# The last stage's first layer in 128 + 128 + 64 rows, with the 64-row products of both column halves on two row tiles

## The reference

```python
def _moe2_ref(x, w_in, w_out, g_ln):
    h = x @ w_in                                   # [1536, 320] @ [320, 1024]
    h_max = np.max(h, axis=-1, keepdims=True)
    e = np.exp(h - h_max)
    sm = e / (np.sum(e, axis=-1, keepdims=True) + 1e-09)
    solu = h * sm
    mu = np.mean(solu, axis=-1, keepdims=True)
    var = np.mean((solu - mu) ** 2, axis=-1, keepdims=True)
    ln = (solu - mu) / np.sqrt(var + 1e-06) * g_ln
    return (ln @ w_out).astype(np.float32)         # [1536, 1024] @ [1024, 320]
```

## Time and profile before

| | us |
|---|---|
| median of three runs | 579.95 (579.08 to 581.56) |
| the profiled execution's own time | 582.91 |
| its span, first to last instruction | 581.2 |
| TensorE busy in it | 538.9 (93%) |
| VectorE busy | 229.0 (39%) |
| ScalarE busy | 134.7 (23%) |
| mean granted TensorE clock | 0.977 |

### The profile page before, as it was taken

How to read it: one execution, slowest core, us unless ns; L and a number is a source line. 1 busy time by engine, 2 the same in 40 slices (tenths; PEclk the granted TensorE clock), 3 DMA queues, 4 the chain that set the end, 5 groups by cost and what they waited for, 6 DMA issues and landing times.

```text
span 581.2 us, 8810 instructions
## 1 busy us (share of the span) xinstructions
PE 538.9 (93%) x2735; PEld 364.8 (63%) x2736; DVE 229.0 (39%) x502; ACT 134.7 (23%) x283; POOL 100.0 (17%) x121
## 2 busy tenths in 40 slices
PE   2699994489999999999999999999998999999996
PEld 2688993366656666666656666666675465565654
DVE  6197886931121213121211212131102656556643
ACT  3435453001111111111111111111111223323222
POOL 2425540121011001100110110010006112213000
PEclk9999998589999999999999999999998999999999
DMA  5957853557777721101100111010062111111100
GB/s 169 285 166 236 240 177 117 182 177 249 235 230 219 224 107 50 38 23 38 50 25 25 50 38 35 26 50 11 23 203 81 34 34 45 56 34 47 33 23 23
DMA packets 32707, 59.68 MB, mean 103 GB/s; under 512 B 5536, under 2 KB 21888, under 8 KB 32560
## 3 DMA queue, kind: packets, MB, share of 16 engines
q1 hardware_dynamic: 24288, 42.28, 23.1%
q0 software_dynamic: 3136, 10.03, 6.2%
q10 hardware_dynamic: 5264, 7.12, 3.5%
HBM read 49.96 MB, written 9.45 MB: 102 GB/s over the span
## 4 chain that ended last, share of the span: by engine, by line
PE 86%; DVE 6%; DMA 3%; issue 2%; ACT 1%; SPq 1%; POOL 0%; DVEq 0%; POOLq 0%; ACTq 0%
PE ps_y L1134 23%; PE ps_a L1113 9%; PE ps_lr L1113 9%; PE ps_y L1185 8%; PE ps_a L1177 6%; PE ps_lr L1177 5%; PE ps_b L1123 5%; PE ps_y L1052 3%; PE ps_lr L1103 3%; PE ps_a L1103 2%; PE ps_t L1090 2%; PE ps_b L1194 2%; PE ps_a L1025 2%; PE ps_b L1034 1%; DMA mb_sb<-m_dram 1%
## 5 line engine op out<-in xcount | busy, mean ns | idle before, releaser
L1134 PE MATMUL ps_y<-w_sb,hT 128*128 x496 | 138.7, 433 | 0.5 <-DVE hT L859 0.5
L859 DVE COPY hT<-ps_b 128x512 f32<-128x512 f32 x86 | 55.4, 686 | 209.4 <-PE ps_b L1123 182.4
L1134 PEld LDWEIGHTS ps_y<-w_sb,hT 128*128 128x128 f32 x496 | 93.1, 190 | 42.8 <-issue 8.4
L475 POOL DMA_INDIRECT xg<-x_dram,token_idx x31 | 29.6, 955 | 245.1 <-PE ps_t L1090 240.2
L1113 PE MATMUL ps_a<-w_sb,xT 128*128 x128 | 57.7, 593 | 0.0
L1185 PE MATMUL ps_y<-wout_sb,hT 128*128 128x320 f32 x192 | 53.9, 433 | 1.9 <-DVE hT L859 1.9
L1113 PE MATMUL ps_lr<-w_sb,xT 128*128 x120 | 55.5, 605 | 0.0
L1185 PEld LDWEIGHTS ps_y<-wout_sb,hT 128*128 128x128 f32 x192 | 35.6, 190 | 16.1 <-DVE hT L859 2.4
L576 ACT COPY y_sb<-ps_y 128x320 f32<-128x320 f32 x31 | 13.2, 426 | 122.7 <-PE ps_y L1134 122.7
L1113 PEld LDWEIGHTS ps_lr<-w_sb,xT 128*128 128x128 f32 x120 | 21.6, 189 | 26.5 <-issue 26.5
L1113 PEld LDWEIGHTS ps_a<-w_sb,xT 128*128 128x128 f32 x128 | 23.1, 190 | 23.3 <-issue 23.3
(11 more groups left out here) (164 smaller groups left out, 559.3 us busy)
## 6 DMA issues: line engine op xcount, KB each, us to landing
w_sb<-w SPq DMA_DIRECT2D x8, 1280.0 KB, 6.2
w_sb<-w SPq DMA_DIRECT2D x16, 512.0 KB, 4.3
mb_sb<-m_dram SPq DMA_DIRECT2D x12, 512.0 KB
y_dram<-y_sb ACTq DMA_DIRECT2D x31, 160.0 KB, 1.8
kvo_sb<-kvo SPq DMA_DIRECT2D x12, 324.0 KB
qk_sb<-qk SPq DMA_DIRECT2D x24, 160.0 KB
w_sb<-w SPq DMA_DIRECT2D x16, 128.0 KB, 5.0
gate_o<-og ACTq DMA_DIRECT2D x1, 1920.0 KB, 7.6
```

The costliest lines, as they stand in the source:

```text
L475: pool.indirect_dma_start(out=xg[:, b % 2], out_offset=None, in_=x_dram, in_offset=bass.IndirectOffsetOnAxis(ap=token_idx[:, b:b + 1], axis=0)
L859: dve.tensor_copy(hT[:, n * 4:n * 4 + 4], ps_b[:, n].rearrange("p (k s) -> p k s", s=P)).then_inc(ready, 1)
L1134: last = pe.matmul(ps_y[:, 0:DM], hT[:, k], w.rearrange("p o n -> p (o n)"), start=(k == 0), stop=(k == FT - 1))
```

## The change

`x2` gets 384 columns, and `combine` writes its last 64 a second time. `turn_rows` makes three transposes of 128 columns (the same that `turn_block` made before, which now calls it), and `copy_xT` copies all 128 partitions. `w_in` is laid out like an expert's first layer, `[128, 5, 512]`: two pieces of 128 rows, each with two column halves, and a last slot whose partitions 0 to 63 hold the last 64 rows for the first half and partitions 64 to 127 the same rows for the second. It is loaded by four DMAs instead of three. `in_layer` does the 64-row products first and then the four products of 128 rows. Stage two is the same but for the shared helpers.

```diff
-        x2 = at("x2", [P, DM], F32, w1_at + 24576)
-        win_sb = at("win_sb", [P, 3, F], F32, w1_at + 28672)
+        x2 = at("x2", [P, DG], F32, w1_at + 24576)
+        win_sb = at("win_sb", [P, W1_TILE, HALF], F32, w1_at + 28672)
...
-            for k, (k0, kn) in enumerate(KT):
-                sp.dma_start(win_sb[0:kn, k], w_in[k0:k0 + kn]).then_inc(win_in, 16)
+            for k in range(KF):
+                sp.dma_start(win_sb[:, 2 * k:2 * k + 2],
+                             w_in[k * P:(k + 1) * P].rearrange("p (a n) -> p a n", a=2)).then_inc(win_in, 16)
+            for n in range(2):
+                sp.dma_start(win_sb[ODD_TAIL * n:ODD_TAIL * (n + 1), 2 * KF],
+                             w_in[TAIL:DM, n * HALF:(n + 1) * HALF]).then_inc(win_in, 16)
...
+            def copy_xT(t, u, turned, ready):
+                dve.wait_ge(turned, done(t))
+                dve.tensor_copy(xT[:, u], ps_t[:, 0:3 * P].rearrange("p (k s) -> p k s", s=P)
+                                ).then_inc(ready, 1)
+
             def copy_block(b, u):
-                dve.wait_ge(b_turned, done(b))
...
+                copy_xT(b, u, b_turned, b_xT)
...
-                dve.scalar_tensor_tensor(out=x2[:], in0=yab[:, u, 1], scalar=top_w[:, 1, ds(t, 1)],
-                                         in1=yab[:, u, 0], op0=ALU.mult, op1=ALU.add).then_inc(s_x2, 1)
+                dve.scalar_tensor_tensor(out=x2[:, 0:DM], in0=yab[:, u, 1], scalar=top_w[:, 1, ds(t, 1)],
+                                         in1=yab[:, u, 0], op0=ALU.mult, op1=ALU.add)
+                dve.scalar_tensor_tensor(out=x2[:, DM:DG], in0=yab[:, u, 1, TAIL:DM],
+                                         scalar=top_w[:, 1, ds(t, 1)], in1=yab[:, u, 0, TAIL:DM],
+                                         op0=ALU.mult, op1=ALU.add).then_inc(s_x2, 1)
...
             def turn_rows(src, turned):
-                for k, (k0, kn) in enumerate(KT):
-                    last = pe.transpose(ps_t[0:KR, k * P:(k + 1) * P], src[:, k0:k0 + KR], ident[:])
+                for k in range(KF + 1):
+                    last = pe.transpose(ps_t[:, k * P:(k + 1) * P], src[:, k * P:(k + 1) * P], ident[:])
                 last.then_inc(turned, 1)
...
-            def tails(b, u):
-
-                pe.wait_ge(expert_here, done(b))
-                pe.wait_ge(b_xT, done(b))
+            def tail_products(hidden, u, weights):
+
                 for q in range(2):
                     for n in range(2):
                         rows = slice(ODD_TAIL * n, ODD_TAIL * (n + 1))
...
+                        last = pe.matmul(hidden[:, n, q * QUART:(q + 1) * QUART], xT[rows, u, KF],
+                                         weights[rows, q * QUART:(q + 1) * QUART], start=(q == 0), stop=False)
+                return last
...
             def in_layer(t, u):
                 pe.wait_ge(s_xT, done(t))
                 pe.wait_ge(s_mean, done(t - R))
+                tail_products(ps_hidden[u], 0, win_sb[:, 2 * KF])
                 for n in range(2):
-                    for k, (k0, kn) in enumerate(KT):
-                        last = pe.matmul(ps_hidden[u][:, n], xT[0:kn, 0, k], win_sb[0:kn, k, n * HALF:(n + 1) * HALF],
-                                         start=(k == 0), stop=(k == 2))
+                    for k in range(KF):
+                        last = pe.matmul(ps_hidden[u][:, n], xT[:, 0, k], win_sb[:, 2 * k + n],
+                                         start=False, stop=(k == KF - 1))
                     last.then_inc(s_hidden, 1)
...
-            pe.wait_ge(win_in, 48)
+            pe.wait_ge(win_in, 64)
```

More of the change, by code:

```diff
@@ L942, in _ @@
             combine(0, 0)
-            copy_xT(0, s_turned, s_xT)
+            copy_xT(0, 0, s_turned, s_xT)
             dve.wait_ge(wout_in, 16)
@@ L948, in _ @@
             combine(1, 1)
-            copy_xT(1, s_turned, s_xT)
+            copy_xT(1, 0, s_turned, s_xT)
             combine(2, 0)
             solu(0, 0)
-            copy_xT(2, s_turned, s_xT)
+            copy_xT(2, 0, s_turned, s_xT)
             copy_vT(0)
@@ L959, in _ @@
                     solu(t, 1 - u)
-                    copy_xT(t + 2, s_turned, s_xT)
+                    copy_xT(t + 2, 0, s_turned, s_xT)
                     copy_vT(t)
@@ L964, in _ @@
             solu(NT - 3, 1)
-            copy_xT(NT - 1, s_turned, s_xT)
+            copy_xT(NT - 1, 0, s_turned, s_xT)
             copy_vT(NT - 3)
@@ L1088, in turn_block @@
                 pe.wait_ge(b_xT, done(b - 1))
-                for k in range(KF + 1):
-                    last = pe.transpose(ps_t[:, k * P:(k + 1) * P], xg[:, u, k * P:(k + 1) * P], ident[:])
-                last.then_inc(b_turned, 1)
+                turn_rows(xg[:, u], b_turned)
             def expert_of(b):
                 return pe.value_load(block_expert[0:1, ds(b, 1)], min_val=0, max_val=E - 1)
+            def tail_products(hidden, u, weights):
+                for q in range(2):
+                    for n in range(2):
+                        rows = slice(ODD_TAIL * n, ODD_TAIL * (n + 1))
+                        last = pe.matmul(hidden[:, n, q * QUART:(q + 1) * QUART], xT[rows, u, KF],
+                                         weights[rows, q * QUART:(q + 1) * QUART], start=(q == 0), stop=False)
+                return last
             def tails(b, u):
@@ L1099, in tails @@
                 pe.wait_ge(b_xT, done(b))
[L1100 to L1105, removed]
+                tail_products(ps_hidden[u], u, tail_sb[:, u]).then_inc(b_tails, 1)
             def first_layer(b, u):
```

## The result

| | before | after |
|---|---|---|
| median, us (7 runs each) | 582.78 (579.08 to 583.54) | 576.35 (574.79 to 578.09) |
| the profiled execution, us | 582.91 | 577.50 |
| its span, us | 581.2 | 575.7 |

The ratio is 0.9891, 95% interval 0.9861 to 0.992: the changed kernel is faster by 1.1%, between 4.7 and 8.1 us. The prediction was 575.0 us in 572.3 to 577.3, a gain of 5.0 us. The kernel before had four more runs beside the changed one, and they raised its median from 579.95 to 582.78; the forecast time was made from the lower one.

The account below looks back on a forecast made before the run. TensorE's program was taken to bound the last stage. Terms of -0.44 (tile 0), +0.05 (tile 1) and -10 x 0.46 us (tiles 2 to 11) gave -5.0, so 579.95 became 575.0 us, range 572.3 to 577.3.

Parts of the forecast that it names:

- The bound: Last stage: TensorE's program sets the time, 10.67 us per tile before, with no idle time in its rows.
- The turn: Last stage, each tile: L1194 to next x2 transposes falls from 6.03 to 5.57 us, saving 0.46; turn 10.21 us.
- The reason for the gaps: Beside the 64-row group on TensorE: gaps of 0.10, 0.21 and 0.10 us belong to changing tile shape, not register loads.
- VectorE: Last stage's loop: one added scalar_tensor_tensor per tile costs 0.20 us (0.16 to 0.26), making the chain 8.77 us.
- Cover: Last stage's loop through VectorE and ScalarE: 1.1 us left before it would delay TensorE.
- Tile 0: Last stage's first tile: first layer takes 6.3 us instead of 6.96, partly at half clock; 0.44 us gained overall.
- Tile 1: Last stage's second tile: VectorE's chain ends last, 6.74 us against 6.73; no gain, 0.05 us cost, TensorE waits about 0.7.
- Transfers: Loading w_in by four DMAs: last landing about 430.4, hidden by 3 us; without cover at most 0.43 us once.
- A free change of shape: Rival, 64-row group on TensorE: shape changes cost nothing, saving 0.86 us a tile, 570.5 us; chance 0.09.
- The loop through VectorE: Rival, last stage: VectorE and ScalarE loop limits the turn to some 10.4 us, gain 0.25 a tile, 577 us; chance 0.07.
- Serial row tiles: Rival, 64-row products: row tiles run one after the other, group 0.86 us longer, kernel 584.5 us; chance 0.03.
- The second stretch at half clock: Rival, start of last stage: TensorE's longer waits bring another half-clock stretch costing 1.7 us, 576.7 us; chance 0.09.

Follow-up runs that it names:

- experiment 1: Changed kernel plus one identity product, between the 64-row pairs or, as control, among full-height products: turn 10.83 against 10.42 us; single times 585.07 and 581.08 us.
- experiment 3: Changed kernel with both column halves' 64-row products on partitions 0 to 63, without the second row tile: 588.16 us, 1.0097 of the kernel before.
- experiment 4: Changed kernel with one memset of 128x800, or two of 128x1000, on VectorE ahead of each combination: single times 581.11 and 583.30 us.
- second copy: The changed kernel run once more with nothing edited: 576.72 us (12 runs), 0.9913 of the kernel before.
- nine unfilled traces: Traces of the changed kernel and its edits without identity products added to fill TensorE's waits at the last stage's start; filling alone took 574.09 us.

## Why the prediction was right, point by point

- **The bound.** TensorE's program sets the last stage before and after: no wait in any of the ten turns. Right.
- **The turn.** Forecast 5.57 and 10.21 us, measured 5.56 and 10.20. Every term was read from the expert stage's rows, and they held: 0.96 (forecast 0.97), 1.07 (1.07), 3.53 (3.53).
- **The reason for the gaps.** Changes of tile shape, as said, shown by experiment 1, and not the pairing of row tiles (experiment 3); the price of one change is 0.2 us, twice what the words gave it, while the sum had both halves.
- **VectorE.** Forecast 0.20 us for the added operation, measured 0.20 from start to start. The loop 8.77 us, as forecast. Cover: forecast 1.1, measured 1.1 by experiment 4. The copy of xT takes 0.55 us in both kernels. Right.
- **Tile 0.** Forecast 6.3 us at a clock that falls once, measured 6.13 in the trace where it did. In the trace of the changed kernel it did not fall, and the layer took 4.60. This is 1.5 to 1.7 us that the forecast did not have, of which tile 1 gave 0.45 back (7.18 against 6.73). It is no merit of the change, since the second copy of the same kernel had the fall.
- **Tile 1.** That its whole gain goes to the chain through VectorE was right: 6.73 us in the second copy's trace against 6.74 forecast. In the changed kernel's own trace it was 7.18, because a gather came last there; this term the forecast lacked. The new wait ahead of tile 0's L1201 was 0.49 in the first of these and 0.94 in the other, around the 0.7 forecast.
- **Transfers.** Hidden, as forecast: TensorE's products on the identity start 433.37 - 428.96 = 4.41 us after the last second layer of the expert stage before, and 434.38 - 429.97 = 4.41 after the change.
- **The sum.** From tile 0's x2 transposes (442.77, before; 441.89, second copy) to the end of the span it is 138.4 us before and 132.8 in the second copy: 5.6 us less, and the 0.20 of the first combination lies ahead of that. That gives 5.4 against the 5.0 forecast; half of the rest is tile 0's layer (0.83 less, not 0.66), half the ten turns (4.75 less, not 4.55). The two timed comparisons, 6.4 us (4.7 to 8.1) and 5.1 us (3.1 to 6.9) less by their ratios, both hold 5.0 and 5.4.
- **The time.** 575.0 forecast, 576.35 measured. This is closer than the forecast earned, since two errors pulled against each other. The start value was 2.8 us too low: the median of before was taken from three runs, 579.95, and is 582.5 to 583.3 over 7 to 17 runs. The timed gain was 6.4 and not 5.0, though 5.0 is within its interval. With the start value of seven runs the same gain gives 582.78 - 5.0 = 577.8 us, which is above the stated range of 572.3 to 577.3 and 1.4 above what was measured. So the turn and the gain were right by their mechanism, and that the time itself fell in the range was in part luck.
- **The rivals.** A free change of shape is ruled out by the turn and by experiment 1. The loop through VectorE needs 1.1 us more (experiment 4). Serial row tiles cost what was said when forced (group 1.92 us, experiment 3). The second stretch at half clock was given too little: of the nine unfilled traces that hold the change, six have stretches at half clock at the start, three of them one and three of them two, at 1.7 us each. The three with two are all of edited kernels (experiments 1, 3 and 4), and the changed kernel as it is had none and one. Whether the change makes a second one more likely is not shown, since the kernel before has one trace, with one stretch.

## What to carry to other kernels

A contraction of 64 rows left over from a cut of 128 is worth putting on two row tiles only if what it saves (here 0.86 us) is more than the two changes of tile shape (0.41 us together); on one row tile it loses. So gather all products of the small shape in one group, and look for the same form elsewhere in the trace first, since its start-to-start distances give the price before anything is built. Where an engine becomes faster, look at the first turns apart: there one tile's gain went into a wait that the steady turns don't have. And take the start value of a forecast from enough runs: here three gave 2.8 us less than seven.

## What was not expected of the hardware

One change of tile shape costs 0.2 us (0.41 for two more, experiment 1), in two halves of 0.1 that stand at the end of one group and at the start of the next; a reading of one side alone gives half the price. Two 64-row products of 512 columns on different row tiles overlap as fully (1.06 us for the group) when one is issued whole ahead of the other as when pieces of 256 take turns (1.07). And the clock at the start of this stage is not a property of the kernel: of two executions of the same program one had a stretch of 3.4 us at 1.2 GHz there and one had none, which by itself moves the time by up to 1.7 us.
